# Attention and two feed-forward layers in one kernel: order of weight loads against the store of kept weights, banks at the phase switch, GpSimd for x's sums in layer 2, and another order in step 0

## The reference

```
kv  = einsum('bhsd,bhse->bhde', k, v)            # 4 batches x 8 heads, 576 tokens, head size 64
out = einsum('bhsd,bhde->bhse', q, kv)
x   = out / sqrt(mean(out*out, -1) + 1e-6) * g_norm     # then (2304 tokens, 512)
h = x @ w_in;  x = (h * sigmoid(1.702*h)) @ w_out       # layer 1, hidden size 2048
h = x @ w_in2; g = max(h,0) + log1p(exp(-|h|))          # layer 2 (softplus)
return g @ w_out2
```

## Time and profile before

| | |
|---|---|
| median of 3 runs | 885.9 us |
| the profiled execution's own time | 886.62 us |
| its span, first to last instruction | 884.8 us |
| TensorE matmul busy | 823.8 us (93%) |
| VectorE busy | 582.3 us (66%) |
| ScalarE busy | 426.9 us (48%) |
| GpSimd busy | 223.1 us (25%) |
| DMA | 139.26 MB, 157 GB/s over the span |

### The profile page before, as it was taken

The page is one execution under the profiler, slowest core; times in us unless marked ns, Lnnn a source line. Parts: engine busy times, 40 slices in busy tenths (PEclk is TensorE's granted clock), DMA queues, the critical chain, the costliest instruction groups (busy, mean ns, idle before and its releaser), DMA issues.

```text
span 884.8 us, 12334 instructions
## 1 busy us (share of the span) xinstructions
PE 823.8 (93%) x4584; PEld 745.7 (84%) x4584; DVE 582.3 (66%) x1024; ACT 426.9 (48%) x814; POOL 223.1 (25%) x262
## 2 busy tenths in 40 slices
PE   6788999999999999797988899998899998899998
PEld 6787999989999989796877788897788897789996
DVE  4567657586556785454477477669676679677674
ACT  4562243233212332212146666766776766676665
POOL 0999777232213102335243322000000000000000
PEclk9998999999999999898988899999999999999999
DMA  9943648224655435453722274232262242263222
GB/s 315 346 184 135 214 178 320 85 107 140 218 198 175 174 115 190 184 178 143 254 80 106 105 264 168 104 147 84 83 212 110 92 159 84 83 194 128 84 84 71
DMA packets 25674, 139.26 MB, mean 157 GB/s; under 512 B 2448, under 2 KB 8208, under 8 KB 18448
## 3 DMA queue, kind: packets, MB, share of 16 engines
q1 hardware_dynamic: 25040, 138.16, 43.5%
q10 hardware_dynamic: 576, 0.33, 0.1%
HBM read 104.40 MB, written 34.08 MB: 157 GB/s over the span
## 4 chain that ended last, share of the span: by engine, by line
PE 71%; DVE 10%; DMA 8%; ACT 5%; issue 3%; POOL 3%; SPq 0%; ACTq 0%; DVEq 0%
PE ps L555 33%; PE ps L610 18%; PE ps L618 11%; PE ps L615 7%; DMA w_kept<-w_in 4%; DVE xs_f L869 2%; DMA w_out_f<-w_out 2%; DVE gs_f L902 1%; DMA kv_in_sb<-k_v 1%; DVE xs L877 1%; DVE ex L933 1%; DVE gs_f L936 1%; DVE gs_f L940 1%; POOL xs L447 1%; ACT gs L741 1%
## 5 line engine op out<-in xcount | busy, mean ns | idle before, releaser
L555 PE MATMUL ps<-xs,w_in 128*128 128x384 f32 x2016 | 419.3, 343 | 40.7 <-DVE gs_f L902 24.7
L555 PEld LDWEIGHTS ps<-xs,w_in 128*128 128x128 f32 x2016 | 362.7, 192 | 72.4 <-issue 25.3
L610 PE MATMUL ps<-w_out,gs 128*128 128x512 f32 x864 | 230.2, 399 | 4.7 <-ACT xy L780 3.6
L902 DVE TENSOR_TENSOR gs_f<-ps,gs_f 128x384 f32<-128x384 f32 x240 | 133.0, 554 | 154.2 <-PE ps L555 153.9
L610 PEld LDWEIGHTS ps<-w_out,gs 128*128 128x128 f32 x864 | 162.3, 190 | 29.9 <-issue 5.8
L618 PE MATMUL ps<-gs,w_out 128*128 128x512 f32 x576 | 149.4, 395 | 0.0
L618 PEld LDWEIGHTS ps<-gs,w_out 128*128 128x128 f32 x576 | 106.6, 189 | 16.6
L412 POOL TENSOR_TENSOR w_in<-w_in_f,w_in 128x256 fp32r<-128x256 f32 x112 | 82.8, 773 | 112.1 <-ACT w_in L746 111.8
L725 ACT ACTIVATE lg<-gs_f 128x384 f32<-128x384 f32 x72 | 37.4, 524 | 126.9 <-DVE gs_f L902 126.9
L615 PE MATMUL ps<-gs,w_out 128*128 128x256 f32 x576 | 87.0, 288 | 0.0
L741 ACT CAST gs<-gs_f 128x384 fp32r<-128x384 f32 x96 | 48.8, 508 | 79.1 <-DVE gs_f L940 78.0
(11 more groups left out here) (59 smaller groups left out, 556.8 us busy)
## 6 DMA issues: line engine op xcount, KB each, us to landing
w_in<-w_kept SPq DMA_DIRECT2D x40, 1792.0 KB, 7.6
w_kept<-w_in SPq DMA_DIRECT2D x16, 1792.0 KB, 12.6
kv_in_sb<-k_v SPq DMA_DIRECT2D x16, 512.0 KB, 9.8
w_in_f<-w_in SPq DMA_DIRECT2D x16, 512.0 KB, 4.1
w_out_f<-w_out SPq DMA_DIRECT2D x16, 512.0 KB, 6.9
q_sb<-q_t SPq DMA_DIRECT2D x16, 288.0 KB, 10.6
out<-xy SPq DMA_DIRECT2D x18, 256.0 KB, 7.8
tail_sb<-k_v SPq DMA_DIRECT2D x3, 256.0 KB, 12.8
```

The source lines that it names most:

```text
L555: mm = nc.tensor.matmul(ps[:, bank, 0:HALF], w[:, wp, W_OF[k], cols], xs[:, k, xp, t], start=(new and t == 0 and (wp, xp) == (HI, HI)), st ...
L610: mm = nc.tensor.matmul(ps[:, ACC_BANK + j, 0:DM], g[:, j * P:(j + 1) * P], w, start=new, stop=done)
L902: nc.vector.tensor_tensor(to, bank, other, ALU.add).then_inc(added, 1)
```

## The change

1. SyncE: at a step after one of `SECOND_AT` the raw load comes first; `load_w_out` comes ahead of `keep`. In the attention the raw loads come at units 1, 4, 8 and the w_out load at 11.
2. ScalarE and GpSimd do w_out ahead of w_in's HI and LO parts.
3. GpSimd prepares all three w_in pairs of the start (`w_all`) before x's sums.
4. `acc_bank`: in layer 2 tile j uses bank (j + 4) % 6, so the tiles that are used first lie in the banks that are copied first; the remaining copies come ahead of `round_g` of the tile before.
5. T1 is made by VectorE in the chunk's last step, rounded by ScalarE ahead of B22 and of `hidden(m, C11)`.
6. For the chunks that begin at steps 32 and 40 (`X_LATE_FROM` = 4) GpSimd makes x's four sums, all seven HI parts and the LO parts of B11 and B21; VectorE keeps five LO parts. The sums lie in buffer 2 of `w_in32`.
7. `gate` is cut in two: in layer 1 the addition U3 stands between C11's product and its split. In step 0 the splits of C11 and C21 come behind the additions that follow them, ScalarE does `hidden(0, C11)` ahead of the last gain, and VectorE makes the first chunk's x sums one unit later.

```diff
-        X_HI_ORDER = (B11, B21, T3, T2, T4, B22, T1)
+        X_HI_ORDER = (B11, B21, T3, T2, T4, T1, B22)
+        X_LATE_FROM = CHUNKS + 1
+        X_LATE_ORDER = (T2, T3, T4, T1, B22)
+        X_LATE_HI_ORDER = (B11, T2, B21, T3, T4, T1, B22)
...
+        def acc_bank(phase, j):
+            return ACC_BANK + (j if phase == 0 else (j + KT) % ACC_BANKS)
...
-            W_AT = {3: 0, 6: 1, 14: 2}
+            W_AT = {1: 0, 4: 1, 8: 2}
...
-                if u == 10:
+                if u == 11:
                     load_w_out(0, 0)
...
             for m in range(ALL):
+                if m - 1 in SECOND_AT and split_at(m - 1) + 1 < 2 * STEPS:
+                    load_raw(split_at(m - 1) + 1)
                 if m + W_BUFS < STEPS:
                     load_raw(m + W_BUFS)
                 if m + 1 < STEPS:
                     keep(m + 1)
                 if STEPS <= m + 2 < ALL:
                     load_operands(m + 2)
+                if m + 2 < STEPS:
+                    load_w_out(m + 2, 0)
+                if SWAP_FROM - 1 <= m < SWAP_FROM - 1 + STEPS:
+                    load_w_out(m - SWAP_FROM + 1, 1)
                 if m == STEPS - 1:
                     load_raw(STEPS)
                 if m in SECOND_AT:
                     keep(split_at(m))
-                    if split_at(m) + 1 < 2 * STEPS:
-                        load_raw(split_at(m) + 1)
-                if m + 2 < STEPS:
-                    load_w_out(m + 2, 0)
-                if SWAP_FROM - 1 <= m < SWAP_FROM - 1 + STEPS:
-                    load_w_out(m - SWAP_FROM + 1, 1)
...
+            def x_late_sum(ci, slot):
+                i = X_RAW_ORDER.index(slot)
+                if i == 0:
+                    if ci == X_LATE_FROM:
+                        pool.wait_ge(w_stored, 16 * 2 * STEPS)
+                    else:
+                        pool.wait_ge(x_split, x_splits(ci - 1, B22))
+                elif slot in (T2, T4):
+                    pool.wait_ge(x_raw_late, 4 * (ci - X_LATE_FROM) + i)
+                a, b, op = x_sum_of(ci, slot)
+                nc.gpsimd.tensor_tensor(x_sum(ci, slot), a, b, op).then_inc(x_raw_late, 1)
+            def x_late(ci, slot):
+                pool.wait_ge(prod_done, PRODUCTS * (STEPS * ci - 1) + slot + 1)
+                if slot == T2:
+                    pool.wait_ge(x_raw_late, 4 * (ci - X_LATE_FROM + 1))
+                nc.gpsimd.tensor_copy(xs[:, slot, HI], x_of(ci, slot)).then_inc(x_hi_late, 1)
+                if slot in (B11, B21):
+                    pool.wait_ge(x_hi_late, 7 * (ci - X_LATE_FROM) + X_LATE_HI_ORDER.index(slot) + 1)
+                    for k in range(KH):
+                        nc.gpsimd.tensor_tensor(xs[:, slot, LO, k], x_of(ci, slot)[:, k],
+                                                xs[:, slot, HI, k].bitcast(F32), ALU.subtract).then_inc(x_split_late, 1)
...
+            w_all(0)
             x_early(B11)
-            w_all(0)
+            w_all(1)
             x_early(B21)
-            w_all(1)
+            w_all(2)
...
             for m in range(1, ALL):
+                ci, p = m // STEPS, m % STEPS
                 d = split_at(m)
                 if d:
                     w_sums(d)
+                if w_out_of(m):
+                    w_out_low(m)
+                if d:
                     pool.wait_ge(w_hi_made, d - W_POOL + 1)
                     w_low(d)
-                if w_out_of(m):
-                    w_out_low(m)
+                if X_LATE_FROM <= ci + 1 < 2 * CHUNKS:
+                    if 4 <= p < STEPS:
+                        x_late_sum(ci + 1, X_RAW_ORDER[p - 4])
+                    if p == STEPS - 1:
+                        for slot in X_LATE_HI_ORDER:
+                            x_late(ci + 1, slot)
...
-                return (3, 4, 5, 6, 1, 2)[j] if m == PHASE1 else j + 1
+                return j + 1
...
             for m in range(ALL):
                 ci, p = m // STEPS, m % STEPS
+                ends = p == STEPS - 1 and ci + 1 < X_LATE_FROM
+                begins = p == 0 and 0 < ci < X_LATE_FROM
                 if m > 0:
                     first_product(m)
+                if p == 1 and ci > 0:
+                    copy_sums(ci - 1, first_copies(ci - 1), ACC_BANKS)
                 if m > PHASE1:
                     round_g(m - 1, C12)
-                if p == 1 and ci > 0:
-                    copy_sums(ci - 1, first_copies(ci - 1), ACC_BANKS)
-                if p == STEPS - 1 and m < ALL - 1:
+                if ends:
                     round_x(ci + 1, B11)
-                hidden(m, C11)
+                if begins:
+                    round_x(ci, T1)
+                    round_x(ci, B22)
+                if m > 0:
+                    hidden(m, C11)
+                if w_out_of(m) and m > 0:
+                    round_w_out(m)
                 if split_at(m):
                     round_w_in(split_at(m))
-                if w_out_of(m) and m > 0:
-                    round_w_out(m)
-                if p == 0 and ci > 0:
-                    round_x(ci, B22)
-                    round_x(ci, T1)
...
-                if u == 2 * PAIRS:
+                if u == 2 * PAIRS + 1:
                     dve.wait_ge(x_made, 2 * PAIRS)
...
-                if m == 0:
-                    add(m, U3)
-                    gate(m, C11)
-                elif phase:
+                if phase:
                     add(m, U3)
                     softplus(m, C11)
+                elif m == 0:
+                    add(m, U3)
+                    gate_product(m, C11)
                 else:
-                    gate(m, C11)
+                    gate_product(m, C11)
                     add(m, U3)
-                if ends:
+                    gate_split(m, C11)
+                if own_sums:
                     low_x(ci + 1, B11)
                     raw_x(ci + 1, T3)
                     raw_x(ci + 1, T2)
-                if begins:
-                    raw_x(ci, T1)
...
                 if ends:
                     low_x(ci + 1, T2)
+                if own_sums:
+                    raw_x(ci + 1, T1)
```

More of the change, by code:

```diff
@@ L252, in x_splits @@
         def x_splits(ci, slot):
-            return 7 * (ci - 1) + X_SPLIT_ORDER.index(slot) + 1
+            if ci < X_LATE_FROM:
+                return 7 * (ci - 1) + X_SPLIT_ORDER.index(slot) + 1
+            return 7 * (X_LATE_FROM - 1) + 5 * (ci - X_LATE_FROM) + X_LATE_ORDER.index(slot) + 1
         def w_out_tile(pair):
@@ L457, in _ @@
             w_out_low(0)
-            w_all(2)
             for m in range(1, ALL):
+                ci, p = m // STEPS, m % STEPS
                 d = split_at(m)
@@ L529, in product @@
                         pe.wait_ge(x_split_early, X_EARLY.index(k) + 1)
+                    elif m // STEPS >= X_LATE_FROM and k in (B11, B21):
+                        pe.wait_ge(x_split_late, 2 * (2 * (m // STEPS - X_LATE_FROM) + (B11, B21).index(k) + 1))
                     else:
@@ L737, in hidden @@
                     nc.scalar.activation(lg[:, i % 2], fix[:, i % 2], ACT.Ln).then_inc(log_made, 1)
+            for u in range(UNITS + TURN_LAG):
+                if u + 1 < UNITS:
+                    copy_kv(u + 1)
+                if u < UNITS:
+                    square(u)
+                if u == UNITS - 1:
+                    first_product(0)
+                if u == UNITS:
+                    nc.scalar.preload_act_table_set("sigmoid_and_others")
+                if u == UNITS + 1:
+                    hidden(0, C11)
+                if u >= TURN_LAG:
+                    gain(u - TURN_LAG)
+                if u < UNITS:
+                    root(u)
             def round_g(m, tile):
@@ L758, in round_x @@
                     act.wait_ge(x_raw_made, x_raws(ci, slot))
-                    x = x_low(slot)
-                else:
-                    x = x_block(ci, 0 if slot == B11 else 1, 1 if slot == B22 else 0)
-                nc.scalar.copy(xs[:, slot, HI], x).then_inc(x_hi_made, 1)
+                nc.scalar.copy(xs[:, slot, HI], x_of(ci, slot)).then_inc(x_hi_made, 1)
             def copy_sums(ci, first, last):
@@ L769, in copy_sums @@
                         act.wait_ge(acc_tile_done, tiles_done(STEPS * ci) + i + 1)
-                        nc.scalar.copy(tile_rows(ci, i), ps[:, ACC_BANK + i].rearrange("p (a n) -> p a n", a=2)
+                        nc.scalar.copy(tile_rows(ci, i), ps[:, acc_bank(1, i)].rearrange("p (a n) -> p a n", a=2)
                                        ).then_inc(acc_copied, 1)
@@ L950, in _ @@
                 ends, begins = p == STEPS - 1 and m < ALL - 1, p == 0 and ci > 0
+                own_sums = ends and ci + 1 < X_LATE_FROM
                 if m > PHASE1:
@@ L978, in _ @@
                 add(m, C21_ADD)
-                if ends:
+                if m == 0:
+                    gate_split(m, C11)
+                if own_sums:
                     raw_x(ci + 1, T4)
@@ L990, in _ @@
                 else:
```

(8 more changed lines are left out.)

70 lines of the change are left out of this document (38 added, 32 removed).

## The result

The changed kernel takes **852.8 us** (median of 4 runs, 852.34 to 856.4) against 885.4; ratio 0.9638, 95% interval 0.9614 to 0.9663. It was faster, as forecast, but by 33 us and not 47: 852.8 lies 0.8 above the range's end of 852 and 14 above the forecast. The profiled execution's own span is 850.9.

What follows compares the result with a forecast made beforehand. TensorE was taken as the bound, quiet steps at 15.73 us. Wins 22.1 + 13.0 + 8.7 - 1.5 + 2.4 + 2.2 = 46.9 off 886.6 gave 839.7, stated as 839; own range 833 to 845, wide range 831 to 852.

Steps and rivals of the forecast that it cites:

- Part 3: Steps 31, 32, 39, 40: x's sums in layer 2 taken off VectorE and ScalarE; win 8.7 us, bounds 3 and 12.
- the sums have three steps' room, the rest fits step 31: Layer 2: GpSimd's added x work, 17 us per chunk, finds room in the steps up to 31.
- I count 0.3 per chunk: Steps 31 and 39: the cost to VectorE of working beside GpSimd's added x work, 0.3 us per chunk.
- Part 2: Phase switch, steps 24 to 31: stalls of 4.37 and 3.61 us shrink or go; win 13.0 us, 4.1 over left.
- Part 1: Steps 18 to 23: SyncE issuing w_out ahead of the store ends three stalls; win 22.1 us, 1.8 over left.
- Part 4: Layer 1's chunk transitions and gate, steps 2 to 17: 5.3 us over where 3.8 was; loss 1.5 us.
- Part 5: The start: step 1 begins near 69.7, win 2.4 us, and the clock stays up there, win 2.2 more.
- rival B: Steps 31 and 39: GpSimd blocks VectorE by whole instructions, 7.4 us over each, some on 23 and 28; 855 us, chance 0.09.
- Rival D: Steps 20, 22, 26: raw load ahead of the operand read becomes the new wait, 16 us beyond; 890 us, chance 0.02.
- Rival C: Steps 18 to 25: w_out still lands too late, 12.0 us after issue, beside the operand read; 849 us, chance 0.08.
- E: Steps 18 to 23: stalls stay because the order of issues is not what ScalarE waits for; 861 us, chance 0.04.
- rival A: Steps 0, 24, 32, 40: remaining waits of 1.5 to 2 us lower the clock, 9 us more; 848 us, chance 0.14.

Runs made afterwards that it cites:

- e12: Changed kernel with GpSimd's late sums of x held by waits, one or two per step, instead of four in a row: 843.6 us in one run.
- e11: Changed kernel with late sums and LO parts of B11 and B21 on VectorE, its list reordered, GpSimd keeping only the roundings: 836.2 us, ratio 0.9423.
- e1: Changed kernel with X_LATE_FROM set to 6, so VectorE and ScalarE prepare x for steps 32 and 40 too: 850.5 us in one run.
- e3: Changed kernel with SyncE's old order again (store, raw load, then w_out): 877.0 us.
- e7: Changed kernel with layer 2's tiles in the old banks and the old table of waits, copies still ahead of the rounding: 858.9 us.
- e8: Changed kernel with both splits of step 0 ahead of the additions again: 854.4 us.
- e5: Control: the changed kernel without any edit, run again: 853.75 us, ratio 0.9621.
- e10: Changed kernel with GpSimd preparing the third w_in pair behind x's sums and w_out again: 857.4 us.
- e2: Changed kernel with the late chunks' four sums of x made by VectorE in a chunk's sixth and seventh step: 846.3 us, ratio 0.9536.
- e4: Changed kernel with each of GpSimd's late sums issued as two instructions of half the columns: 854.1 us.

## Why the prediction was wrong

**Part 3 failed, at the sentence "the sums have three steps' room, the rest fits step 31".** I had read from the list that one sum stands in each of steps 28 to 31 and so charged nothing for them. The trace shows them in a row. Against e12 they cost 4.6 us up to step 31 and 4.7 from 32 on: 9.3 of the 13.0 us between the forecast span (839.7 - 1.8 = 837.9) and the measured one. Half of it is waiting, nearly all of the rest the lower clock in steps 29 and 33, which the forecast had charged nowhere in layer 2.

The second error is in the sentence "I count 0.3 per chunk". The LO parts and roundings made P7 of 31 and 39 wait 1.24, and steps 31 and 32, and 39 and 40, were 4.9 over in each pair without the sums, against 2.7: 4.3 us in all. e11 took the LO parts off GpSimd and gained 2.2 per pair. Part 2 missed 1.0 us, and parts 1, 4 and 5 together came out 1.7 better than forecast, which closes the sum to 0.1. Of the 8.7 us that part 3 was to win in steps 32 to 46 it won 1.5 (e1's 14.0 over against 12.5).

Its mechanism stood in rival B, in its full form. What B had wrong is the place: it put the price at steps 31 and 39, 7.4 each, where it was 2.2 above my sum, and hardly any at 28 and 33. It also rests on 13.6 us of VectorE's own work in step 31, which the traces do not give: the 25 instructions that begin in that step before the change last 16.2 us in all, and less the five that left (0.95 each) that makes 11.5. That B's number, 855, was the nearest of all is luck, a sum of two errors. (Rival D's 16 us three times make 887, not 890.)

**The port.** A VectorE instruction with two SBUF operands took 2.04 to 2.21 us beside sums of 2.0 to 2.15, 1.26 to 1.37 beside halves, and the one that reads a bank 0.54. The Trainium skill's page "SBUF — State Buffer", section "Who interferes with whom", says that a VectorE instruction with two SBUF inputs contends with a GpSimd instruction that reads SBUF, and that the shared port pair is an exclusive lock. The runs agree. I had that rule and used it as an all-or-nothing rival instead of asking, for every GpSimd instruction that was added, what VectorE does at that moment.

**Part 1 was right**, mechanism and size: 1.2 over for 1.8, w_out landing 8.1 us after issue in the median (about 8 taken), ScalarE's longest wait for it 2.8. Rival C falls with these numbers, D with the operand read that went out as early as before, E with e3.

**Part 2 was right in kind.** No wait for copies at 25. P5 of 24 waits 1.94, not 1.4, because C11's `low_g` still loses time beside GpSimd's w_out work, which the forecast had taken as gone:

```profile
445.49 3.45 POOL L473 TENSOR_TENSOR w_out<-w_out_f,w_out 128x256 fp32r<-128x256 f32 x4 [10.38 <-ACT w_out L827]
```

```profile
447.22 1.13 DVE L1020 TENSOR_TENSOR gs<-gs_f,gs 128x384 fp32r<-128x384 f32 x1 [0.58 <-ACT gs L816]
```

At its usual 0.56 the wait would be about 1.4, by my estimate. Steps 24 to 27 are 67.85 - 62.92 = 4.9 over for 3.9 forecast. What the forecast laid to the banks was theirs for 1.6 us only (e7).

**Part 4** was right in sum, 5.7 for 5.5: P3 of step 7 waits 1.51 for the 1.1 forecast, P5 of 8 and 16 1.05 as said.

**Part 5** had the size and the wrong reason. Step 1 began 3.7 us earlier (2.4 forecast): 1.3 because step 0 itself began earlier, which varies by 1.6 us among the profiles, and 2.4 in step 0. "Now the additions go first" is worth nothing there (e8), and which piece won the 2.4 stays open. The clock in step 1, which I expected to stay up, stayed up in six of the thirteen profiles of these variants. So rival A was right in part: with the same idle time of 1.92 to 2.03 in it, step 24 took 18.6 us at a granted clock of 1.00 in nine of the thirteen and 19.9 at 0.91 in four. The sentence "no clock loss, since no idle time here is above 2 us" therefore does not hold in each execution: a wait of 1.67 ahead of step 29 was followed by 0.90 in e5 and by 1.00 in e7.

## What to carry to other kernels

Where an instruction stands in an engine's list is not when it runs: work with no wait on the step runs as soon as its data is there, and a burst of it can fall on the busiest neighbour. Before giving GpSimd work that VectorE has no time for, look which of VectorE's instructions read two SBUF operands meanwhile (in e10 a rounding copy with one operand was held too, 1.72 us). Each can wait for a whole GpSimd instruction. Hold GpSimd's instructions with one more wait until VectorE is idle (e12), or leave the work on VectorE (e2, e11); making them shorter shortened the single wait (e4), but showed no gain in time. Count for a stall on TensorE also the slower matmuls that may follow. In a queue that runs in order, put nothing that another engine needs soon behind a wait for a store that has only just been issued.
